# Expert units of up to 448 rows in place of two-tile and one-tile units

## The reference, cut to what matters

```python
def _moe_ref(x, w_skip, w_gate, w1, w2):
    do_compute = (x @ w_skip) > 0
    out = x.copy()
    xc = x[do_compute]
    logits = xc @ w_gate
    e_idx = np.argmax(logits, axis=1)
    ...
    for e in range(E):
        mask = e_idx == e
        h = np.maximum(xc[mask] @ w1[e], 0.0)
        y[mask] = gate_w[mask, None] * (h @ w2[e])
    out[do_compute] = xc + y
```

## Time and profile before

| | us |
|---|---|
| median of three runs | 616.67 (616.22 to 620.47) |
| the profiled execution | 612.81 |
| its span | 611.1 |
| TensorE busy in the span | 561.2 (92%) |
| VectorE busy | 401.2 (66%) |
| GpSimd busy | 309.3 (51%) |
| ScalarE busy | 248.6 (41%) |

### The profile page before, as it was taken

One profiled execution on the slowest core, in us unless ns is written; L12 is line 12 of the kernel. 1 busy time (PEld: TensorE's weight loads), 2 busy tenths in 40 slices (PEclk: granted clock), 3 DMA queues, 4 the chain that ended last, 5 costly groups with the idle time before them and its releaser, 6 DMA issues. The chain is left out here.

```text
span 611.1 us, 17083 instructions
## 1 busy us (share of the span) xinstructions
PE 561.2 (92%) x5997; PEld 540.8 (88%) x5998; DVE 401.2 (66%) x787; ACT 248.6 (41%) x629; POOL 309.3 (51%) x378
## 2 busy tenths in 40 slices
PE   3999999978799999999938889999999999999993
PEld 2899899967699999999936779999999999999993
DVE  5888888859668777777814835664766755738331
ACT  0233333334256665555504044633464624425321
POOL 5877777830556676666610054443535534525321
PEclk9899999998899999999979899999999999999998
DMA  9788899675576666776178017070617161111100
GB/s 142 111 179 160 165 166 167 133 250 203 178 235 193 197 195 222 244 235 190 44 223 314 1 50 246 31 257 26 222 67 257 26 246 36 39 36 32 49 27 13
DMA packets 113728, 88.78 MB, mean 145 GB/s; under 512 B 80475, under 2 KB 104724, under 8 KB 113680
## 3 DMA queue, kind: packets, MB, share of 16 engines
q1 hardware_dynamic: 106304, 74.16, 42.6%
q0 software_dynamic: 7376, 14.03, 8.8%
HBM read 79.06 MB, written 13.57 MB: 152 GB/s over the span
## 5 line engine op out<-in xcount | busy, mean ns | idle before, releaser
L789 DVE TENSOR_TENSOR w_lo<-w_raw,w_hi 128x384 fp32r<-128x384 f32 (+1 forms) x164 | 132.8, 837 | 2.0 <-issue 1.2
L1040 PE MATMUL e_ps_y<-w_hi,hidden 128*128 128x384 f32 x344 | 119.7, 348 | 0.0
L1042 PE MATMUL e_ps_y<-w_hi,hidden 128*128 128x384 f32 x344 | 115.3, 335 | 0.0
L1041 PE MATMUL e_ps_y<-w_lo,hidden 128*128 128x384 f32 x344 | 115.2, 335 | 0.0
L784 ACT CAST w_hi<-w_raw 128x384 fp32r<-128x384 f32 (+1 forms) x224 | 114.4, 558 | 0.5
L789 POOL TENSOR_TENSOR w_lo<-w_raw,w_hi 128x512 fp32r<-128x512 f32 (+1 forms) x60 | 79.9, 1355 | 26.4 <-ACT w_hi L784 26.1
L1124 ACT CAST e_x_hi<-e_ps_x 128x384 fp32r<-128x384 f32 x47 | 22.6, 481 | 113.2 <-PE e_ps_x L1024 106.7
L1040 PE MATMUL e_ps_h<-e_x_hi,w_hi 128*128 128x256 f32 x228 | 64.9, 285 | 3.4 <-DVE e_x_lo L1188 3.4
L956 POOL DMA_INDIRECT rows<-x_rows,e_ent_in x45 | 48.2, 1072 | 37.9 <-POOL e_ent_in L952 37.0
L1042 PE MATMUL e_ps_h<-e_x_hi,w_lo 128*128 128x256 f32 x228 | 65.0, 285 | 0.0
L1041 PEld LDWEIGHTS e_ps_y<-w_lo,hidden 128*128 128x128 f32 x344 | 64.9, 189 | 0.0
(11 more groups left out here) (164 smaller groups left out, 1199.3 us busy)
## 6 DMA issues: line engine op xcount, KB each, us to landing
w_raw<-in_moe_w_dram SPq DMA_DIRECT2D x32, 1536.0 KB, 7.2
r_in<-in_r_dram SPq DMA_DIRECT2D x24, 192.0 KB, 3.2
k_in<-in_k_dram SPq DMA_DIRECT2D x24, 192.0 KB, 3.9
v_in<-in_v_dram SPq DMA_DIRECT2D x24, 192.0 KB, 3.9
x_rows<-rows SPq DMA_DIRECT2D x24, 192.0 KB, 3.5
w_lo<-x_rows SPq DMA_DIRECT2D x6, 768.0 KB, 7.6
rows<-x_rows,e_ent_in POOLq DMA_INDIRECT x45
out_dram<-rows,e_ent_out POOLq DMA_INDIRECT x17
```

The source lines that it names most:

```text
L789: eng.tensor_tensor(self._of(self.lo1[par], self.lo2[par], n), self._of(self.raw1[par], self.raw2[par], n), self._of(self.hi1[par], self.h ...
L1040: pe.matmul(o, s_hi, m_hi, start=(k == 0), stop=False)
L1041: pe.matmul(o, s_hi, m_lo, start=False, stop=False)
L1042: return pe.matmul(o, s_lo, m_hi, start=False, stop=(k == last))
```

## The change

`WIDTHS` names two unit widths for each layer: full and last. In the first layer an expert has full units of 256 rows and a last one of 256 or 208; in the second, full units of 384 and a last one of 384 or 448. An expert of the first layer with at most 208 rows is one unit of 208, and one of the second with more than 384 and at most 448 is one unit of 448. So with the counts above the first layer has eight units of 208 in place of eight `two`, and the second has five units of 384 (in place of a `two` and a `one`) and three of 448 (in place of two `two`). The form `one` is gone, with its transposes.

Every unit has the form of `two`. Its down phase has a block of 24 multiplies for each tile; the last tile of a 208 or 448 unit has 80 or 64 rows. X tiles are turned for the next unit at fixed places (`turns`): two in the first layer, always four in the second. Gathers go to X row buffers with a semaphore each; the copy `take` is gone. `y_rows` has four buffers. `route` counts against a list of limits in place of a shift, `table` has 53 columns, 45 of them placed by the products, and `starts` also holds where the full units end. `row_hot` has a tensor of its own.

```diff
--- before
+++ after
+WIDTHS = ((256, 208), (384, 448))
...
+        FULL, LAST = WIDTHS[m]
+        MOST = TILES * P // FULL
+        TALL = FULL // P
+        LIMITS = TALL * MOST
...
-        row_hot = hot[:, 0:TILES * P].rearrange("p (i r) -> p i r", r=P)
+        row_hot = sb("row_hot", [P, TILES, P])
...
+                one, two = slice(TALL, TALL + MOST - 1), slice(TALL + MOST - 1, LIMITS)
+                pool.iota(limit[:, one], [[FULL, MOST - 1]], base=FULL, channel_multiplier=0, **exact).then_inc(limits_made, 1)
+                pool.iota(limit[:, two], [[FULL, MOST - 1], [0, 2]], base=LAST, channel_multiplier=0, **exact).then_inc(limits_made, 1)
...
-            link(dve.tensor_scalar(cnt_i[:], seen[:, :, TILES - 1], float(P - 1), None, ALU.add))
-            link(dve.tensor_scalar(cnt_i[:], cnt_i[:], 7, None, ALU.logical_shift_right))
-            link(dve.tensor_scalar(n_tiles[:], cnt_i[:], 1.0, None, ALU.max))
+            count = seen[:, :, TILES - 1:TILES].to_broadcast([P, E, LIMITS])
+            dve.wait_ge(limits_made, 3 if m == 0 else 6)
+            link(dve.tensor_tensor(over[:], count, limit[:].unsqueeze(1).to_broadcast([P, E, LIMITS]), ALU.is_gt))
+            link(dve.tensor_reduce(n_tiles[:], over[:], AX.X, ALU.add))
...
+            if m == 0:
+                link(dve.tensor_tensor(over[:], count, of_full[:].unsqueeze(1).to_broadcast([P, E, LIMITS]), ALU.is_gt))
+            else:
+                link(dve.tensor_tensor(over[:], over[:], of_full[:].unsqueeze(1).to_broadcast([P, E, LIMITS]), ALU.mult))
+            link(dve.tensor_reduce(full[:], over[:], AX.X, ALU.add))
+            dve.tensor_tensor(starts[:, E + 2:2 * E + 2], base[:], full[:], ALU.add)
+            dve.tensor_copy(starts[:, 2 * E + 2:2 * E + 3], base[:, 0:1])
...
-    QF = 256
-    Q = F // QF
-    KQ = QF // P
+    FULL, LAST = WIDTHS[m]
+    X = -(-LAST // P) if m else 2
+    XW = LAST if m else FULL
...
-        x_hi = sb("x_hi", [P, DC, 2 * P], F32R)
-        x_lo = sb("x_lo", [P, DC, 2 * P], F32R)
-        h_row = sb("h_row", [P, F])
...
+        x_hi = sb("x_hi", [P, DC, XW], F32R)
+        x_lo = sb("x_lo", [P, DC, XW], F32R)
+        h_hi = sb("h_hi", [P, FC, XW], F32R)
+        h_lo = sb("h_lo", [P, FC, XW], F32R)
...
+        def units_once(pe, ep, par, unit):
+
+            lo, mid, hi = tiles_of(pe)
+            load_ahead(pe, 2 * ep + par)
+            with pe.If(lo < mid):
+                with pe.Fori(lo, mid, FULL // P) as t:
+                    unit(t, FULL)
+                    unit_done(pe)
+            with pe.If(mid < hi):
+                unit(mid, LAST)
+                unit_done(pe)
+            next_span(pe)
+
+        def tiles(width):
+            return [slice(t0, min(t0 + P, width)) for t0 in range(0, width, P)]
+
...
+            for n in range(X):
+                pool.indirect_dma_start(x_in[n][:], None, rows, bass.IndirectOffsetOnAxis(ap=table[:, n, 0:1], axis=0),
+                                        bounds_check=bound, oob_is_err=False).then_inc(gathered[n], 16)
...
-
-                def ahead(t):
-
-                    pool.wait_ge(x_taken, t)
-                    gather(t)
-
-                def send(t, tiles):
-
-                    pool.wait_ge(scattered, 16 * (t + 1))
-                    for slot in range(tiles):
-                        entries(t + slot, slot)
-                    for slot in range(tiles):
-                        scatter(t + slot + 1, slot)
-
-                def two(t, pieces, midway):
-                    ahead(t + 3)
+                def unit(t, width, pieces, midway):
+                    u = unit_of(pool)
+                    parts = tiles(width)
+                    if m == 1:
+                        pool.wait_ge(x_turned, X * u + X)
+                        for n in range(X):
+                            gather(t + len(parts) + n, n, X * u + n + 1)
                     midway()
                     for n in pieces:
-                        split(n)
-                    ahead(t + 4)
-                    send(t, 2)
-
-                def one(t, pieces, midway):
-                    ahead(t + 3)
-                    midway()
-                    for n in pieces:
-                        split(n)
-                    send(t, 1)
-                units(pool, ep, par, W.pool_pieces if nxt else [], two, one)
+                        W.lo(pool, pairs * m + ep + par, 1 - par, n)
+                    if m == 0:
+                        for n in range(X):
+                            pool.wait_ge(x_turned, X * u + X + n + 1)
+                            gather(t + 2 * X + n, n, X * u + X + n + 1)
+                    pool.wait_ge(scattered, 16 * (t + 1))
+                    for slot in range(len(parts)):
+                        entries(t + slot, slot)
+                    for slot, rows_of in enumerate(parts):
+                        scatter(t + slot + 1, slot, rows_of.stop - rows_of.start)
...
-            def turn_x(t, slot, src=x_row):
-
-                pe.wait_ge(x_taken, t + 1)
+            def turn_x(unit, n):
+
+                pe.wait_ge(gathered[n], 16 * unit + 16)
+                if not isinstance(unit, int) or n >= 2:
+                    pe.wait_ge(x_lo_done, X * unit + n - 1)
                 for c in range(DC):
-                    ins = pe.transpose(ps_x[slot][:, P * c:P * c + P], src[:, P * c:P * c + P], ident[:])
+                    ins = pe.transpose(ps_x[n % 2][:, P * c:P * c + P], x_in[n][:, P * c:P * c + P], ident[:])
                 ins.then_inc(x_turned, 1)
 
             stay_warm(pe, ident, ps_y[0][:, 0:P], 3)
-            pe.wait_ge(first_in, 16)
-            turn_x(0, 0)
-            stay_warm(pe, ident, ps_y[0][:, 0:P], 1)
-            pe.wait_ge(second_in, 16)
-            turn_x(1, 1, y_rows[0])
+            for n in range(X):
+                turn_x(0, n)
...
-                def two(t):
+                def unit(t, width):
+                    u = unit_of(pe)
+                    parts = tiles(width)
+                    w = slice(0, width)
+                    turns = {(0, 1): 0, (0, 5): 1, (1, 1): 2, (1, 5): 3}
 
                     W.wait_split(pe, 0, pairs * m + ep, par)
-                    pe.wait_ge(x_lo_done, t + 3)
-                    pe.wait_ge(x_hi_moved, t + 1)
-                    pe.wait_ge(x_lo_moved, t + 1)
+                    pe.wait_ge(x_lo_done, X * u + len(parts))
                     for k in range(FC):
                         if k >= 4:
 
-                            pe.wait_ge(h_lo_done, 4 * t + k - 1)
+                            pe.wait_ge(h_lo_done, FC * u + k - 3)
                         f = slice(P * k, P * k + P)
                         for c in range(DC):
-                            ins = product(ps_c[k % 4][:, 0:2 * P], (hi1[:, c, f], lo1[:, c, f]), (x_hi[:, c, :], x_lo[:, c, :]), c, DC - 1)
+                            ins = product(ps_h[k % 4][:, w], (hi1[:, c, f], lo1[:, c, f]), (x_hi[:, c, w], x_lo[:, c, w]), c, DC - 1)
                         ins.then_inc(h_ready, 1)
 
                     W.wait_split(pe, 1, pairs * m + ep, par)
-                    pe.wait_ge(y_done, t + 1)
-                    for n in range(2):
+                    for n, rows_of in enumerate(parts):
+
+                        pe.wait_ge(y_done, t + max(n, 1))
+                        o = ps_y[n % 2][0:rows_of.stop - rows_of.start, 0:D]
                         for k in range(FC):
                             if n == 0:
 
-                                pe.wait_ge(h_lo_done, 4 * t + k + 3)
-                            if k == FC // 2:
-                                turn_x(t + 2 + n, n)
-                            ins = product(ps_y[n][:, 0:D], (h_hi[:, k, SLOT[n]], h_lo[:, k, SLOT[n]]), (hi2[:, k, :], lo2[:, k, :]), k, FC - 1)
-                            if n == 1 and k == 0:
-
-                                ins.then_inc(h_turned, 2 * Q)
+                                pe.wait_ge(h_lo_done, FC * u + k + 1)
+                            if turns.get((n, k), X) < X:
+                                turn_x(u + 1, turns[n, k])
+                            ins = product(o, (h_hi[:, k, rows_of], h_lo[:, k, rows_of]), (hi2[:, k, :], lo2[:, k, :]), k, FC - 1)
                         ins.then_inc(y_ready, 1)
-
...
+                        if m == 1 or k % 4:
+                            between()
...
-                        if k % 2 or k == FC - 2:
+                        if k % 2 if m == 0 else 0 < k < FC - 1:
                             between()
...
-                    result(t, 0)
-                    take(t + 3)
-                units(dve, ep, par, W.dve_pieces if nxt else [], two, one)
+                    for n, rows_of in enumerate(parts):
+                        result(t, n, rows_of.stop - rows_of.start)
+                        if n == 0:
+                            for later in range(2, X):
+                                x_low(u + 1, later)
+                            while left:
```

(7 more changed lines are left out.)

344 lines of the change are left out of this document (135 added, 209 removed).

## The result

The changed kernel takes **631.43 us** (median of 4, 630.63 to 632.64) where the kernel before takes 617.04 in the same comparison (616.22 to 620.47): a ratio of 1.021, 95% interval 1.016 to 1.027. (Ratios leave disturbed runs out, so they can differ a little from the quotient of two medians.) I had forecast 604, at most 614, so this is a slowdown of 14 us in place of a gain of 12.5. The profiled execution has a span of 630.8 us against 611.1, 19.7 us more, and that difference is what has to be found. It is larger than the 14 us of the medians: the kernel before was profiled in an execution of 612.81 us, under the 616.22 to 620.47 of the comparison, and the changed kernel in its longest, 632.64. So some 5 of the 19.7 us belong to the choice of executions, and where they lie no kept trace shows.

A forecast was written before the change was run, and what follows sets the result against it. PE was taken to bound both expert layers. Terms -14.0 - 4.2 + 2.8 + 1.2 + 1.7 = -12.5 us gave 600.3 from the profiled 612.8; taken from the median 616.67, the forecast was 604, range 594 to 614.

The forecast's parts named there:

- Second layer's units, -14.0: Second layer: five 384-row units at 26.3 us and three 448-row at 32.4 make 228.7 us against 242.5.
- PE bound: Both expert layers: time goes where PE's stream goes, as long as the other engines keep up; chance 0.58.
- First layer, -4.2: First layer: 576 multiplies shrink from 256 to 208 columns, 0.1199 to a floor of 0.1126 us each.
- Routing, +2.8: Routing of both layers: larger and additional DVE operations cost 1.9 us in the first layer, 0.9 in the second.
- Second layer's start, +1.2: Before the second layer's first unit: PE must turn four tiles, the fourth by 360.0 against 358.85 us.
- Clock, +1.7: Second layer's start: one stretch of lower granted clock, charged as in the first layer's first unit, 1.7 us lost.
- Hidden: Both layers: GpSimd's gathers fit beside PE's work, at most 9 of 26 us in a second-layer unit, costing nothing.
- Rival B: Second layer: weight pieces before VectorE's last blocks make PE wait 1 to 2 us per unit, 616; 0.18 with other lateness.
- A: Rival, first layer: 208-column multiplies reach 0.0997 us and the clock holds, giving 595 us; chance 0.15.
- C: Rival, first layer: 208-column f32r multiplies run at the plain f32 rate, 0.344 us each, +129 us, 733; chance 0.08.
- D: Rival, first layer: widths don't fit the row counts, an expert over 208 rows costing +0.5 us each; chance 0.01.
- The chance of 0.09 for slower: Whole kernel: probability given to a slower result, beside 0.76 faster and 0.15 the same; same reached up to 622.8 us.

The follow-up runs named there:

- kernel 13: Changed kernel without 256-row code in the first layer, later weight loads, last two experts looped, plus throw-away TensorE transposes at both layers' starts: 611.51 us, ratio 0.992.
- kernel 14: Changed kernel without 256-row first-layer code, later weight loads, last two experts looped, plus GpSimd's first-layer scatters ahead of gathers: 623.49 us, ratio 1.011.
- kernels 3, 5 and 6: Changed kernel with: weight loads issued later, 620.66 us; only TensorE jumping in the first layer, 629.35; that with the layer's first loads later, 623.14.

## Why the prediction was wrong

- **Second layer's units, -14.0: right for steady units.** Five times 26.37 and three times 32.68 are 229.9 us, 12.9 below the 242.8 of before. (228.7 - 242.5 is -13.8; I had written -14.0.) The 448-column step was 0.203, not 0.200. But the layer took 251.4, **21.5 us more than eight steady units**, and most of that was spent in first passes, a term that the sum does not have. The step that failed is the one behind "PE bound": I priced each of the eight units by a steady one, because before, the first was no dearer than the rest. The same step failed at the first layer's start (+6.4). Of the 21.5, PE's idle time is 12.2 us: 10.4 of it the three stops of 2.46, 5.96 and 1.97 at late code, 1.3 the two waits of 0.66 and 0.61 for VectorE's long pieces. Low clock is 6.9 (PE's busy time times one less the granted clock, summed over windows of 2 us); before, both are nil. 2.4 us are left.
- **First layer, -4.2: right in mechanism.** 0.1115 us a multiply against my floor of 0.1126, seven periods 3.9 us shorter. The Trainium skill's formula ("TensorE: Matmul & The Clock Gate", "Back-to-back issue gap") gives 0.089. The section has it for an isolated multiply and says that it comes out too low at few columns in a stream of loads and multiplies, which my prediction left out; the trace of the changed kernel agrees with that, 0.1115. What was left of this layer, +6.4 at its start, was not in the sum.
- **Routing, +2.8:** 2.1. The first layer's 1.9 came exactly, the second's 0.9 was 0.2.
- **Second layer's start, +1.2:** 3.3. PE starts the fourth turn 7.97 us after its first warming transpose (358.74 to 366.71), where the second came after 5.23 (351.48 to 356.71): 2.7 of the 3.3. I had the gathers 1.4 us apart and right, but not that each of the later turns took 0.90 us at the lower clock against 0.55, nor what the waits added.
- **Clock, +1.7:** I charged one new low stretch, in the second layer; there were four. In the first layer 2.9 us were lost, not 1.7; keeping PE busy (kernel 13) removes it there.
- **"Hidden":** GpSimd's gathers most likely were not: at the passage nothing follows that could hide them. It grew by 1.8 us; that the gathers are the cause is argued only (kernel 14).
- **Rival B, VectorE late:** its mechanism is real and its size was wrong. The pieces ahead of the last blocks made PE wait twice, 0.66 and 0.61 us, not 1 to 2 us in each of eight units; a piece lasted 4.5 us there, where I had allowed 0.99. It isn't a matter of first passes: in kernel 13 the fourth and the eighth expert run the same code, and the wait comes both times (0.66, 0.68). The 2.46 us was VectorE's own late code. **A** and **C** are refuted by 0.1115, **D** by the sequence of widths (384, 448, 384, 384, 448, 448, 384, 384).
- The chance of 0.09 for slower had no mechanism of the right kind behind it. The change itself showed it: the `LAST` unit stands behind a `FULL` one. The Trainium skill says what that does, in "Runtime: NRT & Kernel Launch", section "Instruction fetch mechanics": fetching runs ahead in sequence only, and a taken branch whose target isn't there yet stalls for the fetch. I read past it. The runs agree: 0.3 us for a jump over one transpose, 3.8 over a unit, 6 with loads in flight, with an instruction packet inside each long stop looked at and none inside the short one. The page gives no price for it, and none for the loads.

What stays open: what holds the instruction packet back by 2 us while loads are in flight (that it queues behind them on the shared DMA engines fits kernels 3, 5 and 6, but no run gave it another way), which first meetings stop an engine and which don't, what stretches VectorE's pieces to 4.5 us beside GpSimd's, and the last 2.4 us of the second layer.

## What to carry to other kernels

Cost a change by its first passes too: count the code that each engine jumps over before it first runs a unit, and put the variant that runs first directly in line, or leave out the one that isn't needed. A first meeting behind a long jump, where it stopped TensorE, cost 4 to 6 us here in most cases (2 to 3 in some), plus 1 to 3 of low clock, and that outweighed the 16 us that the narrower units saved over both layers. Don't start bulk loads at the moment when an engine enters new code; here a wait of a few microseconds on the loads cost nothing that shows, and gave back 6.5.
